# A two-resolution attention and two wide layers on one core: high halves moved later, the denominator's constant added by a sum over pairs, a new order at the attention's end, and VectorE's inverse first in each period

## What is computed

```python
def _attn_ref(q, k, v):                       # 4 batches, 8 heads, 576 rows, 64 columns
    q_d, k_d, v_d = (t.reshape(B, H, S // 4, 4, D).mean(axis=3) for t in (q, k, v))
    out_up = np.repeat(sm_attn(q_d, k_d, v_d), 4, axis=2)      # sm_attn: softmax(q k' / 8) v
    mask = np.abs(pos[:, None] - pos[None, :]) < 4
    scores = np.where(mask, scale * np.matmul(q, k.transpose(0, 1, 3, 2)), -1e9)
    attn = np.exp(scores - np.max(scores, axis=-1, keepdims=True))
    attn = attn / (np.sum(attn, axis=-1, keepdims=True) + 1e-09)
    return out_up + np.matmul(attn, v)
...
x = attn_out.transpose(0, 2, 1, 3).reshape(2304, 512)
h = x @ w_in;  x = (h - np.tanh(h)) @ w_out                    # 512 -> 2048 -> 512
x = (1 / (1 + np.exp(-(x @ w_gate))) * (x @ w_val)) @ w_out2   # 512 -> 1536 -> 512
```

## Time and profile before

| | us |
|---|---|
| median of 3 runs | 940.01 (939.84 to 942.81) |
| the profiled execution, its own time | 939.61 |
| its span | 937.8 |
| TensorE busy | 898.9 (96%) |
| VectorE, ScalarE, GpSimd busy | 594.8, 386.9, 291.7 |
| attention, until the last of the exponentials | about 118 |

### The profile page before, as it was taken

One profiled execution on the slowest core, in us unless ns is written; L12 is line 12 of the kernel. 1 busy time (PEld: TensorE's weight loads), 2 busy tenths in 40 slices (PEclk: granted clock), 3 DMA queues, 4 the chain that ended last, 5 costly groups with the idle time before them and its releaser, 6 DMA issues.

```text
span 937.8 us, 15651 instructions
## 1 busy us (share of the span) xinstructions
PE 898.9 (96%) x6056; PEld 843.5 (90%) x6056; DVE 594.8 (63%) x918; ACT 386.9 (41%) x752; POOL 291.7 (31%) x237
## 2 busy tenths in 40 slices
PE   7879789999999999999998999999999999999997
PEld 5657679999999999999997999999999999999996
DVE  8779966767865657765668556566544456544444
ACT  4667664535432325332343544454222234222221
POOL 5687866683103000120016555732200001000000
PEclk9889888999999999999999999999999999999999
DMA  9867638568554546464421767779775555565511
GB/s 248 220 157 230 182 113 327 210 262 303 211 207 164 211 160 210 160 214 158 168 91 45 284 262 278 281 287 362 284 282 211 213 210 210 198 274 202 202 45 68
DMA packets 46089, 197.01 MB, mean 210 GB/s; under 512 B 3936, under 2 KB 15552, under 8 KB 33216
## 3 DMA queue, kind: packets, MB, share of 16 engines
q1 hardware_dynamic: 41984, 166.66, 49.4%
q0 software_dynamic: 4032, 29.36, 8.3%
HBM read 139.90 MB, written 56.10 MB: 209 GB/s over the span
## 4 chain that ended last, share of the span: by engine, by line
PE 84%; DVE 6%; POOL 4%; issue 3%; ACT 2%; DVEq 0%; ACTq 0%; POOLq 0%
PE banks L826 45%; PE banks L896 19%; PE banks L1012 16%; PE banks L804 1%; PE banks L781 1%; POOL prob L587 1%; DVE row_den L1342 1%; DVE qk_down L1327 1%; DVE row_max L1308 1%; PE banks L759 1%; DVE x_op L1360 1%; DVE row_sum L1334 1%; POOL v_four L580 1%; PE banks L817 1%; POOL prob_d L587 0%
## 5 line engine op out<-in xcount | busy, mean ns | idle before, releaser
L826 PE MATMUL banks<-x_op,pair 128*128 128x384 f32 x1512 | 278.5, 336 | 1.7 <-DVE cg_sum L1529 1.7
L826 PEld LDWEIGHTS banks<-x_op,pair 128*128 128x128 f32 x1512 | 266.7, 189 | 9.7 <-DVE cg_sum L1529 2.1
L896 PE MATMUL banks<-g_parts,mid 128*128 128x384 f32 x1152 | 227.8, 336 | 5.3 <-DVE x_all L1442 5.2
L896 PEld LDWEIGHTS banks<-g_parts,mid 128*128 128x128 f32 x1152 | 203.4, 189 | 7.1 <-DVE x_all L1442 7.1
L826 PE MATMUL banks<-x_op,win 128*128 128x384 f32 x1008 | 205.3, 340 | 2.7 <-ACT c_sum L1120 2.7
L826 PEld LDWEIGHTS banks<-x_op,win 128*128 128x128 f32 x1008 | 180.6, 192 | 3.6 <-ACT c_sum L1120 3.1
L1012 PE MATMUL banks<-wout,p_parts 128*128 128x512 f32 x648 | 163.6, 393 | 1.7 <-issue 1.7
L1442 DVE TENSOR_TENSOR x_all<-banks,x_all 128x384 f32<-128x384 f32 x168 | 92.8, 555 | 77.3 <-PE banks L896 76.7
L1012 PEld LDWEIGHTS banks<-wout,p_parts 128*128 128x128 f32 x648 | 120.2, 188 | 22.6 <-issue 2.1
L1554 DVE TENSOR_TENSOR x_all<-banks,x_all 128x512 f32<-128x512 f32 x90 | 62.1, 690 | 113.7 <-PE banks L1012 113.7
L1134 ACT ACTIVATE banks<-c_sum 128x384 f32<-128x384 f32 x72 | 35.2, 490 | 94.9 <-DVE c_sum L1409 49.2
(11 more groups left out here) (96 smaller groups left out, 1016.2 us busy)
## 6 DMA issues: line engine op xcount, KB each, us to landing
pair<-kept_pair SPq DMA_DIRECT2D x24, 1792.0 KB, 10.9
win<-kept_in SPq DMA_DIRECT2D x16, 1792.0 KB, 7.4
kept_pair<-pair SPq DMA_DIRECT2D x12, 1792.0 KB, 11.8
mid<-kept_mid POOLq DMA_DIRECT2D x16, 1024.0 KB, 5.1
kept_in<-win SPq DMA_DIRECT2D x7, 1792.0 KB, 5.8
wout<-kept_out POOLq DMA_DIRECT2D x12, 1024.0 KB, 11.8
kept_mid<-mid SPq DMA_DIRECT2D x7, 1024.0 KB, 6.8
kept_out<-wout SPq DMA_DIRECT2D x6, 1024.0 KB, 14.5
```

The costliest lines, as they stand in the source:

```text
L826: mm = pe.matmul(bk[:, 0:T], weights[:, w, p - 1, kk, :], x_op[:, p - 1, x, kk, :], start=(first and kk == 0 and a == 0), stop=(last and k ...
L896: mm = pe.matmul(bk[:, 0:T], w[:, wp, f, m * P:(m + 1) * P], g[:, gp, 2 * f + t, :], start=(f == 0 and a == 0), stop=(f == 1 and a == 2))
```

## The change

- VectorE's `inverses(t-1)` moves to the head of period t, ahead of `local_max(t)`. `row_den` is no longer row_sum plus a constant: row_sum has two columns for each row (the second one holds 1e-9) and a reduction adds each pair.
- The high halves of chunks 0 and 1 move from periods 3, 4 and 7, 8 to 4, 5 and 10, 11; `plain_high(0)` from 6 to 7. GpSimd's `first_weight_low` goes from periods 5 to 8 to 6 to 9, its sums for chunk 1 to periods 5, 7 and 8, `plain_low(0)` to 10. The early stores follow.
- `x_high` and `x_low` of inputs 1, 7 and 6 are spread over periods 12 to 15.
- At the end, product (0,1) goes ahead of the last but one `turn_rest`, and the waits for the last exponentials go to product (0,7). `weight_high(2)` and `plain_high(1)` go from before the first tanh to behind `copy_c(1, C21)`. `second_weight_low` goes ahead of the first `add_c`, the last `write_x` behind the last `g_tile` of n = 0, and GpSimd's `x_last_sum(0)` between two pairs of sums.

```diff
-                if 8 <= u < 12:
-                    keep_early(kept_in[0], flat_f32(win[0][:, :, :, :, :]), s_wlo, lows(0), u - 8)
...
+                if 10 <= u < 14:
+                    keep_early(kept_in[0], flat_f32(win[0][:, :, :, :, :]), s_wlo, lows(0), u - 10)
+                if 11 <= u < 15:
+                    keep_early(kept_mid[0], flat_f32(mid[0][:, :, :, :]), s_mlo, 1, u - 11)
...
-                if 5 <= t < 9:
-                    first_weight_low(t - 5)
-                if t == 6:
+                if t == 5:
                     weight_sums(1, (0, 1))
-                if t == 7:
-                    weight_sums(1, (2, 3))
-                if t == 9:
+                if 6 <= t < 10:
+                    first_weight_low(t - 6)
+                if 7 <= t < 9:
+                    weight_sums(1, (t - 5,))
+                if t == 10:
                     plain_low(0)
...
-            weight_sums(2)
+            weight_sums(2, (0, 1))
             x_last_sum(0)
+            weight_sums(2, (2, 3))
...
+                if t == UNITS - 1:
+                    first_product(0, 1)
...
-                if t == UNITS + 1:
-
-                    act.wait_ge(s_vd, UNITS)
-                    weight_high(2)
-                    plain_high(1)
...
-                if 3 <= t < 5:
-                    half_weight_high(0, t - 3)
-                if 7 <= t < 9:
-                    half_weight_high(1, t - 7)
-                if t == 6:
+                if 4 <= t < 6:
+                    half_weight_high(0, t - 4)
+                if 10 <= t < 12:
+                    half_weight_high(1, t - 10)
+                if t == 7:
                     plain_high(0)
-                if t == 13:
-                    x_high(0, 1)
-                    x_high(0, 7)
+                if 12 <= t < 15:
+                    x_high(0, (1, 7, 6)[t - 12])
...
-                dve.tensor_scalar(row_den[:, :], row_sum[:, :], EPS, None, ALU.add).then_inc(s_den, 1)
+                dve.tensor_reduce(row_den[:, :], row_sum[:, :, :], AX_X, ALU.add).then_inc(s_den, 1)
...
+            dve.memset(row_sum[:, :, 1], EPS).then_inc(s_cols, 1)
...
             for t in range(UNITS + 1):
+                if t >= 1:
+                    inverses(t - 1)
                 if t < UNITS:
                     local_max(t)
                     shift_local(t)
                     down_max(t)
-                if t >= 1:
-                    inverses(t - 1)
```

More of the change, by code:

```diff
@@ L192, in attention_and_mlps @@
         neg_max = low.tile("neg_max", [P, 4])
-        row_sum = low.tile("row_sum", [P, COLS])
+        row_sum = low.tile("row_sum", [P, COLS, 2])
         row_den = low.tile("row_den", [P, COLS])
@@ L857, in first_product @@
                 elif p == 7:
+                    if n == 0:
+                        pe.wait_ge(s_exd, 4 * UNITS)
                     mm = product(c, w, p, True, False)
@@ L925, in _ @@
                 if t == UNITS:
-                    first_product(0, 1)
                     first_product(0, 7)
@@ L1143, in g_high, with first_quad @@
                 act.activation(g_parts[n % 2][:, 0, pick, :], c_sum[n % 2][:, pick, :], ACT.Copy).then_inc(s_ghi, 1)
-            def first_quad(n, skip=0):
+            def first_quad(n):
                 last, s = n % Q1 == Q1 - 1, n // Q1 + 1
-                first = n % Q1 == 0 and n > 0
+                first = n % Q1 == 0
                 if n > 1:
                     g_high(n - 1, 1)
-                if skip < 1:
                     copy_c(n, C11)
-                if n == 1:
-                    g_high(0, 1)
                 if last:
@@ L1158, in first_quad @@
                     x_high(s - 1, 4)
-                if skip < 2:
+                if n > 1:
                     copy_c(n, C22)
@@ L1164, in first_quad @@
                     x_high(s - 1, 3)
-                if skip < 3:
+                if n > 1:
                     copy_c(n, C21)
@@ L1179, in first_quad @@
                 tanh(n, C12)
-                if 1 <= n and n + 1 < Q1:
+                if n + 1 < Q1:
                     plain_high(n + 1)
@@ L1189, in _ @@
                     copy_rest(t - 2, 1)
+                if t == UNITS:
+                    copy_c(0, C11)
+                    x_high(0, 2)
+                    x_high(0, 5)
                 if t == UNITS + 1:
                     x_high(0, 4)
+                    tanh(0, C11)
                 if t < UNITS:
@@ L1203, in _ @@
                     exp_down(t)
-                if 3 <= t < 5:
-                    half_weight_high(0, t - 3)
-                if 7 <= t < 9:
-                    half_weight_high(1, t - 7)
-                if t == 6:
+                if 4 <= t < 6:
[3 more added lines that the diff above has]
+                if t == 7:
                     plain_high(0)
-                if t == 13:
-                    x_high(0, 1)
-                    x_high(0, 7)
+                if 12 <= t < 15:
+                    x_high(0, (1, 7, 6)[t - 12])
                 if t == UNITS:
-                    x_high(0, 6)
-                    x_high(0, 2)
-                    x_high(0, 5)
-                    copy_c(0, C11)
                     x_high(0, 3)
@@ L1224, in _ @@
                     copy_c(0, C21)
-            first_quad(0, skip=3)
+            tanh(0, C22)
+            tanh(0, C21)
+            g_high(0, 0)
+            tanh(0, C12)
+            copy_c(1, C11)
+            g_high(0, 1)
+            copy_c(1, C22)
+            copy_c(1, C21)
+            act.wait_ge(s_vd, UNITS)
+            weight_high(2)
+            plain_high(1)
             for n in range(1, N1):
@@ L1333, in local_sum @@
                 wait(dve, s_den, u)
-                dve.tensor_reduce(row_sum[:, 0:2 * SLOTS], prob[u % 3][:, 0:PROBS].rearrange("p (n c) -> p n c", n=2 * SLOTS), AX_X,
+                dve.tensor_reduce(row_sum[:, 0:2 * SLOTS, 0], prob[u % 3][:, 0:PROBS].rearrange("p (n c) -> p n c", n=2 * SLOTS), AX_X,
                                   ALU.add).then_inc(s_sum, 1)
@@ L1382, in _ @@
                     down_max(t)
-                if t >= 1:
-                    inverses(t - 1)
                 if t + 1 < UNITS:
                     averages(t + 1)
-                if t == 13:
-                    x_low(0, 1)
-                    x_low(0, 7)
+                if 13 <= t < 15:
+                    x_low(0, (1, 7)[t - 13])
                 if t < UNITS:
@@ L1392, in _ @@
                 if t == UNITS:
-                    x_low(0, 6)
+                    x_low(0, 2)
+                    x_low(0, 5)
                 if t >= 2:
                     write_x(t - 2)
-            x_low(0, 2)
-            x_low(0, 5)
+                if t == UNITS - 1:
+                    x_low(0, 6)
             x_low(0, 3)
-            x_low(0, 4)
             def add_c(n, i):
@@ L1470, in first_quad @@
                 add_c(n, C22)
-                if n == 0:
-                    second_weight_low()
-                    write_x(UNITS - 1)
                 g_tile(n, C11)
@@ L1487, in first_quad @@
                     x_low(s, 2)
-            for n in range(N1):
+            second_weight_low()
+            x_low(0, 4)
+            add_c(0, C11)
+            add_c(0, C22)
+            g_tile(0, C11)
+            add_c(0, C21)
+            g_tile(0, C22)
+            g_tile(0, C21)
+            g_low(0, 0)
+            g_tile(0, C12)
+            write_x(UNITS - 1)
+            for n in range(1, N1):
                 first_quad(n)
```

10 lines of the change are left out of this document (3 added, 7 removed).

## The result

| | us |
|---|---|
| before, median of 4 runs | 940.40 (939.84 to 942.81) |
| after, median of 4 runs | 933.29 (928.46 to 935.37) |
| ratio | 0.990, 95% interval 0.9865 to 0.9934 |
| the profiled execution of after, its span | 935.37, 933.6 |

The change makes the kernel faster, by 7 us and not by 18. The forecast of 922 and its range up to 929 are too low.

A forecast was written before the change was run, and what follows sets the result against it. TensorE, busy 96%, was taken as the bound, with gains left in the attention. Attention 71.6 plus 40.1 up to product (2,6) made 111.7 against 129.3, 17.6 us less: 922 us, range 911 to 929.

The forecast's parts named there:

- mark 3: ScalarE's last read of unit 3's exponential sums in the attention; forecast to stay at 27.3 us.
- the stretch: Attention from unit 3's to unit 15's last read of exponential sums on ScalarE; forecast 71.6 us against 90.6 before.
- part 2: From unit 15's last read of exponential sums to the start of product (2,6); forecast 40.1 us against 38.7 before.
- its own bounds, 77 and 43 us: Upper ends: attention 77 us if GpSimd or the reduction is dearer, then 43 us up to product (2,6).
- the sum of part 1: Attention, units 3 to 15: twelve periods at 5.45 us (65.4), plus 3.9 and 2.3, giving 71.6 us.
- 3.9 + 2.3: Added attention work: 3.9 us for ScalarE's put-in halves, 2.3 for two VectorE `x_low` in periods 13 and 14.
- What is late next is GpSimd: Attention: GpSimd, busy 70.8 of 71.5 us, is covered by the earlier `inverses`; 1 to 4 us if not.
- Nothing there waits for a moved step: Attention's start: the first four units were assumed to keep their times, ending at 27.3 us.
- the rival of 3%: Slower: uneven periods leave TensorE at its lower clock through the attention; 24.4 us more, 946 us, chance 3%.
- The wait took the place of the old one: After the attention: ScalarE waits for weight sums and mid_raw, so TensorE stands about 8 us before product (2,6).
- the third part: New order at the attention's end: 40.1 us up to product (2,6) forecast, against 38.7 before.
- the attention not smooth: Rival: attention periods stay at 6.2 us through GpSimd's pace or `row_den` waits; 9 us more, 931, chance 12%.

The follow-up runs named there:

- after_noloads: The changed kernel with q, k and both forms of v loaded for the first buffers only; median 923.9 us, ratio to before 0.9783 to 0.9836.
- after_nov: The changed kernel without the loads of v's windows for units 2 to 15; median 929.4 us, ratio to before 0.9838 to 0.9914.
- after_again: The changed kernel once more, unchanged, for a second measurement and profile; median 930.2 us, ratio to before 0.9855 to 0.9912.
- after_sums6: The changed kernel with GpSimd's weight sums of chunk 1 one step each in periods 6 to 9; median 931.5 us.
- after_swap: The changed kernel with the requests for raw chunk 1 of w_in and raw chunk 0 of mid exchanged, periods 2 and 4; median 931.5 us.
- a_inverse: The kernel before with VectorE's part alone: inverses first in the period, constant added as a sum over pairs; median 934.4 us.
- after_ab: The changed kernel with the new attention periods but before's order at the attention's end; median 926.2 us, ratio to before 0.9810 to 0.9867.
- b_putin: The kernel before with only the attention's put-in work (high and low halves, weight sums, early stores, x_high, x_low) in its new periods; median 929.9 us.

## Why the prediction was wrong, point by point

Against the profiled execution, 935.4 where 922.0 was forecast, the difference of 13.4 is: mark 3 at 29.7 instead of 27.3, 2.4; the stretch 82.1 instead of 71.6, 10.5; part 2 41.2 instead of 40.1, 1.1; the rest of the span 780.6 instead of 781.2, -0.6. The range was also summed too low at its upper end: its own bounds, 77 and 43 us, are 8.3 us above the sum and give 930, not 929. The median of 933.3 is outside either.

- **Right: what goes, and what a period then costs.** The waits for GpSimd's sums are gone. The new reduction of `row_den` takes 0.18 us (0.2 was taken) and is never stretched, as in the row below. Without loads the sum of part 1 comes out within 0.3 us, and that is in part luck. In `after_noloads` three periods take 5.3 us and nine take 5.95 to 6.8: as terms that is 63.6 for the twelve, where 65.4 was taken, and 7.7 for what is added, where 3.9 + 2.3 was.

```profile
11.27 0.18 DVE L1350 TENSOR_REDUCE row_den<-row_sum 128x14 f32<-128x28 f32 x1
```

- **Wrong: the loads stand in the sum with nothing.** "What is late next is GpSimd" named one resource and stopped. Without the unit loads the stretch is 71.3 us, with them 77.6 and 82.1, so they are the term that is missing, 6 to 11 us; GpSimd, which was named, is late mostly because it waits for them. The trace of before could have warned. It moved 196 GB/s for 90.6 us, that is 17.8 MB. In 71.6 us this is 248 GB/s. But where all DMA engines were full in before, they carried 230, as its window from 10 to 28 us shows; in another they carried more:

```profile
10.00:28.00 18.00, 14.71 (x267) 11.40 (x268) 17.31 (x26) 12.37 (x46) 13.35 (x13) 0.91 1.00 230
82.00:95.00 13.00, 10.95 (x220) 8.80 (x221) 12.86 (x19) 9.18 (x32) 11.50 (x11) 1.00 0.90 264
```

At 230 GB/s the same bytes take 77 us, an estimate. With that term the forecast would have been 927 to 928, still below the medians of 930.2 and 933.3. It is a warning and no bound: the second row has 264 GB/s, and `after_nov`, with 13.8 MB in it (173 GB/s for 79.9 us), took 79.9 where 60 would follow. The share of 0.71 looked like a reserve of 29%, and it was an average over stretches with 1.0 and with 0.5. The Trainium skill ("DMA: Bandwidth & Descriptors", "Bandwidth") gives 341 GB/s for a transfer of 1 MB. By that figure the 17.8 MB would take 52 us, an estimate, and the loads would have been no limit. The loads here are mostly of 245 to 512 KB, many at a time, and the trace of after has 213 GB/s for them, at a share of 0.94.
- **Wrong: the first four units unchanged.** "Nothing there waits for a moved step", but moving `inverses` shortens these periods too, and unit 3 then waits 1.60 us for v_win, at the low clock after it. In `after_again` mark 3 is at 26.6, so this term swings by 3 us between two executions of the same kernel, and no forecast from one profile could fix it.
- **Missed: a sum can be too early.** GpSimd's sums of chunk 1 moved from period 6 to 5, ahead of the landing of their chunk: 5.7 to 6.1 us of wait. I had looked only at who waits for the sums, not at what the sums wait for. What it costs isn't shown: `after_sums6` and `after_swap` are without it and no faster.
- **Missed: what a wait costs behind itself.** Where TensorE waited or stood for 1 to 4 us, the period mostly had 0.6 to 0.8 of full clock, and one or two periods take 7.4 to 13 us, the wait included, instead of 5.3 to 6.1. In `after_again` it kept the full clock behind 2.76 us. I had counted this at the end of the attention, and inside only in the rival of 3%. Its source was misread: units 7 to 8 of before did not begin on the lower clock, which was 1.00 from 56.7 to 58.4 us and 0.50 only behind the wait of 5.46 us.
- **Right but for sizes: part 2.** The wait took the place of the old one, where it was said: ScalarE 6.12 us for the sums of chunk 3 and 2.26 for mid_raw, TensorE 6.7 us ahead of block (0,4) (8 forecast), then 5.2 us for three groups instead of 3.1, 2.1 lost (2.0). The landing was at +37.1 (35.9). Reckoned back by its 13 groups, product (1,6) came at +18.8 and not +16.7. Two `x_low` ahead of it took 6.2 us together, beside GpSimd (below), and the prediction had reckoned them out of the chain; that they are what made the product late was not tried.

```profile
115.19 6.22 DVE L1368 TENSOR_TENSOR x_op<-x_all,x_op 128x768 fp32r<-128x768 f32 x2 [1.83 <-ACT x_op L1117]
```

- **Wrong: what this part costs.** I compared 40.1 with the 38.7 of before and had the third part at 1.4. It costs 4. With before's order and another attention ahead of it the same way takes 35.4 us (`a_inverse`, `after_ab`) to 38.4 (`b_putin`), and the 18 matmuls behind TensorE's wait of 2.7 us lose 0.6 to 3.0 us there; 38.7 was the upper end of that.

Of the rivals, the one that came nearest in time (931, the attention not smooth) is also half right in cause: in `after_again` GpSimd sets the pace in the last six periods, 6.5 us each. Without the loads it does so too, but at 5.9 us each.

## What to carry to other kernels

Before counting a stretch as shorter, work out the rate that its bytes would then need and hold it against the rates that the DMA engines reached where they were full; a mean share below 1 is no reserve, and a rate near those is a reason to widen the range. When work is moved to an earlier place, look at its inputs as well as at its users. And where two resources are near full, a wait that is taken away at one of them can come back at the other: here six single changes, four to loads and sums and two to the new end, brought nothing that can be told from noise, and leaving the end as it was brought 4 us.

## What was unexpected of the hardware

- TensorE can stand 2 to 4 us between two matmuls of one block with no semaphore in it, only in kernels with the unit loads, and always at one of a row of places that lie 124 matmuls apart in its list.
- The rate of full DMA engines varied. Of the periods of after, those above have 220 GB/s at a share of 1.00 and 236 at 0.95; these two have 189 and 257:

```profile
37.16:44.27 7.11, 5.62 (x105) 4.18 (x103) 5.52 (x8) 5.34 (x18) 3.92 (x4) 0.91 1.05 189
...
87.86:93.93 6.07, 5.55 (x111) 4.25 (x109) 5.42 (x8) 5.35 (x18) 5.93 (x6) 1.00 1.02 257
```

- The same kernel had the full clock through the whole stretch in one execution (1.00, 77.6 us) and 0.90 in another (82.1 us). The clock can also fall without a long wait: in `after_noloads`, where the longest wait of TensorE in the period was 0.62 us and the DMA engines were idle, two periods had less than 0.9 of it, and the second took 6.8 us instead of 5.3.

```profile
50.43:56.60 6.17, 5.55 (x104) 4.08 (x101) 5.81 (x9) 5.45 (x18) 6.03 (x7) 0.86 0.01 4
56.60:63.40 6.80, 6.80 (x119) 5.39 (x116) 5.57 (x8) 4.60 (x16) 6.66 (x8) 0.88 0.01 4
```
